# First batch's attention outputs held as fp32 and scaled in the second, and the first loads in another order

## What is computed

```python
# q, k, v: (4, 8, 576, 64)
scores = q @ k.T / 8
mask_local   = (rel >= 0) & (rel < 32)                       # heads 0 to 3
mask_strided = (rel >= 0) & (pos_k % 32 == pos_q % 32)       # heads 4 to 7
attn = softmax(where(mask, scores, -1e9))
x = (attn @ v) as (2304, 512)
h = x @ w_in; g = h * sigmoid(1.702 * h); x = g @ w_out      # 512 -> 2048 -> 512
# then a top-2 mixture of 8 experts (512 -> 1024 -> 512) with noisy gates
```

## Time and profile before

| | us |
|---|---|
| median of 3 runs | 1031.27 |
| lowest, highest | 1027.51, 1045.26 |
| the profiled execution's own time | 1028.2 |
| its span in the trace | 1026.4 |
| TensorE busy | 978.1 (95%) |
| VectorE busy | 594.5 (58%) |
| ScalarE busy | 307.6 (30%) |

### The profile page before, as it was taken

The page is one execution under the profiler, slowest core; times in us unless marked ns, Lnnn a source line. Parts: engine busy times, 40 slices in busy tenths (PEclk is TensorE's granted clock), DMA queues, the critical chain, the costliest instruction groups (busy, mean ns, idle before and its releaser), DMA issues.

```text
span 1026.4 us, 22946 instructions
## 1 busy us (share of the span) xinstructions
PE 978.1 (95%) x9218; PEld 706.8 (69%) x9219; DVE 594.5 (58%) x1033; ACT 307.6 (30%) x427; POOL 219.8 (21%) x274
## 2 busy tenths in 40 slices
PE   7899999999999999999999899989999999999992
PEld 4677777867677576775765767756777767677771
DVE  6588998668777786787887744232232323233231
ACT  2355745523243233332531321111111111111110
POOL 4222323000000000010025124233323333333331
PEclk8699999999999999999999999999999999999997
DMA  9774582097756667567647635848474747475330
GB/s 267 177 187 92 129 196 55 6 393 237 249 204 205 247 214 258 181 205 268 219 149 238 218 78 151 263 114 213 131 210 121 221 120 214 133 209 142 89 82 23
DMA packets 170240, 182.43 MB, mean 178 GB/s; under 512 B 133495, under 2 KB 133495, under 8 KB 167360
## 3 DMA queue, kind: packets, MB, share of 16 engines
q1 hardware_dynamic: 112832, 142.47, 44.6%
q0 software_dynamic: 9600, 27.69, 8.9%
q10 hardware_dynamic: 47744, 11.35, 6.3%
HBM read 116.41 MB, written 53.55 MB: 166 GB/s over the span
## 4 chain that ended last, share of the span: by engine, by line
PE 86%; DVE 4%; DMA 2%; SPq 2%; ACT 2%; issue 1%; POOLq 0%; DVEq 0%; ACTq 0%
PE bank L1760 20%; PE bank L1769 20%; PE bank L1661 18%; PE bank L1586 17%; PE bank L1524 4%; PE bank L1562 3%; PE bank L1494 2%; PE bank L1536 1%; PE bank L1543 1%; PE bank L1513 1%; DMA arena<-out,arena 1%; DMA arena<-in_moe_w 1%; DVE sc L976 1%; SPq L399 1%; ACT arena L725 1%
## 5 line engine op out<-in xcount | busy, mean ns | idle before, releaser
L1586 PE MATMUL bank<-x,w_in_s 128*128 128x256 f16 (+1 forms) x1728 | 194.1, 273 | 2.6 <-DVE x L1021 1.5
L1661 PE MATMUL bank<-w_out_s,arena 128*128 128x512 f16 x864 | 190.2, 379 | 0.0
L1586 PEld LDWEIGHTS bank<-x,w_in_s 128*128 128x128 f16 x1728 | 167.9, 98 | 25.9 <-DVE x L1021 1.8
L1661 PEld LDWEIGHTS bank<-w_out_s,arena 128*128 128x128 f16 x864 | 83.6, 98 | 96.6
L1429 DVE TENSOR_TENSOR arena<-arena 128x512 f32<-128x512 f32 x37 | 25.6, 692 | 161.7 <-ACT arena L899 117.6
L1760 PEld LDWEIGHTS bank<-arena,w_out_s 128*128 128x128 f16 x2016 | 114.5, 98 | 5.9 <-issue 0.8
L1760 PE MATMUL bank<-arena,w_out_s 128*128 128x128 f16 x2016 | 117.0, 219 | 0.6 <-issue 0.6
L1760 PEld LDWEIGHTS bank<-arena,w_in_s 128*128 128x128 f16 x1920 | 109.3, 98 | 5.4 <-issue 0.7
L1760 PE MATMUL bank<-arena,w_in_s 128*128 128x128 f16 x1920 | 111.7, 219 | 0.5 <-issue 0.5
L1769 PE MATMUL bank<-w_out_s,arena 128*128 128x512 f16 x480 | 108.7, 383 | 3.3 <-DVE arena L1424 3.3
L1769 PE MATMUL bank<-w_in_s,arena 128*128 128x512 f16 x480 | 108.6, 383 | 2.3 <-DVE arena L1424 2.3
(11 more groups left out here) (196 smaller groups left out, 992.8 us busy)
## 6 DMA issues: line engine op xcount, KB each, us to landing
arena<-in_moe_w SPq DMA_DIRECT2D x16, 2048.0 KB, 11.5
split_weights<-arena SPq DMA_DIRECT2D x16, 2048.0 KB, 7.4
w_in_s<-split_weights SPq DMA_DIRECT2D x32, 512.0 KB
w_out_s<-split_weights SPq DMA_DIRECT2D x32, 512.0 KB
arena<-in_q SPq DMA_DIRECT2D x32, 144.0 KB, 3.6
arena<-in_k SPq DMA_DIRECT2D x32, 144.0 KB, 3.7
out<-zeros SPq DMA_DIRECT2D x1, 4608.0 KB, 25.1
x_rows<-arena SPq DMA_DIRECT2D x18, 256.0 KB, 3.3
```

What stands on the lines that cost most here:

```text
L1586: last = mm(dst, w_in_s[:, w_part, c, f * P:(f + 1) * P], x1[:, x_part, c, tok], start=(c == 0 and w_part + x_part == 0), stop=(c == DC - ...
L1661: last = mm(ps_x[j], g[par][:, g_part, f, j * P:(j + 1) * P], w_out_s[:, w_part, f], start=(n == 0), stop=(n == 3 * FC - 1))
```

## The change

The outputs of batch 0 are written by `out_hi` as unscaled fp32 into `held_out`, space of `x1` that batches 2 and 3 fill later; DVE has no `out_lo` in stages 0 to 3. In stages 4 to 7 ScalarE and DVE each do one more operation a stage, on 128x576, that scales and splits the held output of the pair with the same hp (`late_hi`, `late_lo`). V's factor is needed in stage 4 instead of stage 0.

Flat V comes in four quarters with a semaphore each: two after the start's first and second transposes, two in SP's iteration 2. `v_max` moves from the start to stages 0, 1 and 2. The V loads of pairs 0 and 1 are started by ScalarE. SP loads q and k of pair i + 2 when pair i's are transposed, and V when pair i - 2's product is done. The maxima of `w_in` are taken in stages 3, 4 and 5 (two in stage 5) instead of 1 to 4, `w_in` is split in stages 7 to 10 instead of 6 to 9, `w_out`'s maxima stay in stages 9 to 12. Between the first transposes and scores stand 14 `busy` products.

```diff
-MAX_IN, SPLIT_IN, MAX_OUT, SPLIT_OUT = 1, 6, 9, 14
+SPLIT_IN, SPLIT_OUT = 7, 14
...
             load_qk(0, 0)
             load_qk(0, 1)
-            sp.dma_start(w_in_s[...], v[0:2] ...).then_inc(S["v_flat_in0"], 16)
-            sp.dma_start(w_out_s[...], v[2:4] ...).then_inc(S["v_flat_in1"], 16)
-            load_v(sp, 0, 0)
-            load_v(sp, 0, 1)
+            sp.wait_ge(S["t_done"], 4)
+            load_qk(0, 2)
+            load_v_flat(0)
+            sp.wait_ge(S["t_done"], 8)
+            load_qk(0, 3)
+            load_v_flat(1)
...
-            for i in range(NPAIR - 2):
-                sp.wait_ge(S["s_done"], i * 2 + 2)
+            for i in range(2, NPAIR - 2):
+                sp.wait_ge(S["t_done"], 8 * i - 2)
                 load_qk((i + 2) // PAIRS, (i + 2) % PAIRS)
+                if i == 2:
+                    for n in (2, 3):
+                        load_v(sp, 0, n)
+                        load_v_flat(n)
+                sp.wait_ge(S["pv_done"], 2 * i - 2)
                 load_v(sp, (i + 2) // PAIRS, (i + 2) % PAIRS)
-                if i < QUARTERS:
+                for n in ([0], [1], [2, 3])[i - 2] if i < 5 else []:
                     c = DC // QUARTERS
-                    wait(sp, S["w_in_in"], 16 * i)
+                    wait(sp, S["w_in_in"], 16 * n)
...
-                n, c = i - SPLIT_IN - 3, FC // QUARTERS
+                n, c = i - SPLIT_IN - 1, FC // QUARTERS
                 if 0 <= n < QUARTERS:
                     sp.wait_ge(S["split_lo"], 2 * n + 2)
                     wait(sp, S["w_out_in"], 16 * n)
...
             def out_hi(b, hp):
                 act.wait_ge(S["pv_done"], i * 2 + 2)
+                if b == 0:
+                    for src, dst in out_views(b, hp, None):
+                        last_op = nc.scalar.activation(dst, src, ACT.Copy)
+                    last_op.then_inc(S["x1_lo"], 1)
+                    return
...
+                if b == 1:
+                    act.wait_ge(S["x1_lo"], 2 + hp)
+                    nc.scalar.activation(x1[:, 0, hp, 0:SEQ], held_out[hp], ACT.Copy, scale=col(S_V)
+                                         ).then_inc(S["late_hi"], 1)
...
             evac_qk(1, 0, 1)
+            load_v(act, 0, 0)
             evac_qk(2, 1, 0)
             evac_qk(3, 1, 1)
             exps(0, 0, 0)
             exps(0, 0, 1)
+            load_v(act, 0, 1)
...
+                if b == 1:
+                    dve.wait_ge(S["late_hi"], hp + 1)
+                    nc.vector.scalar_tensor_tensor(x1[:, 1, hp, 0:SEQ], held_out[hp], col(S_V), x1[:, 0, hp, 0:SEQ],
+                                                   ALU.mult, ALU.subtract).then_inc(S["late_lo"], 1)
...
-            ALL_OF = {0: V_ALL, 1: WG_ALL, MAX_IN + QUARTERS: WI_ALL, MAX_OUT + QUARTERS: WO_ALL}
+            ALL_OF = {PAIRS: V_ALL, SPLIT_IN - 1: WI_ALL, 2 * PAIRS + 2: WG_ALL, SPLIT_OUT - 1: WO_ALL}
...
             transpose_qk(1, 0, 1, 16 * QK_DMAS)
+            busy(2)
             pe.wait_ge(S["consts_pool"], 10)
             scores(0, 0, 0, 2)
+            busy(2)
             scores(0, 0, 1, 2)
+            busy(2)
             transpose_qk(2, 1, 0, 16 * QK_DMAS)
             transpose_qk(3, 1, 1, 16 * QK_DMAS)
+            busy(2)
             scores(0, 1, 0, 4)
+            busy(2)
             scores(0, 1, 1, 4)
+            busy(4)
...
-                        scores(b2, hp2, 0, k[2] + 1,
-                               (V_MAX, 1) if hp == 0 else (B_MAX, b + 2) if hp == 1 else None)
+                        scores(b2, hp2, 0, k[2] + 1, spread)
```

More of the change, by code:

```diff
@@ L312, in program @@
         w_ready = [S["w_even"], S["w_odd"]]
+        v_flat = [t[:].rearrange("p a c f -> p (a c f)").bitcast(F32)[:, 0:HEADS * SEQ] for t in (w_in_s, w_out_s)]
+        held_out = [x1[:, 0, hp, 2 * SEQ:4 * SEQ].bitcast(F32) for hp in range(PAIRS)]
         def is_local(hp):
@@ L337, in out_views @@
         def out_views(b, hp, part):
-            tok = slice(b * SEQ, (b + 1) * SEQ) if isinstance(b, int) else bass.ds(b * SEQ, SEQ)
-            dst = x1[:, part, hp, tok]
+            dst = held_out[hp] if part is None else x1[:, part, hp, b * SEQ:(b + 1) * SEQ]
             if is_local(hp):
@@ L401, in load_qk, with load_v_flat @@
                                      ).then_inc(qk_in[par], 16)
+            def load_v_flat(n):
+                half = HEADS * SEQ // 2
+                at = slice(n % 2 * half, (n % 2 + 1) * half)
+                rows = v[n // 2 * 2:n // 2 * 2 + 2].rearrange("b h (x s) d -> (b h x) (s d)", x=P // (2 * HEADS))
+                sp.dma_start(v_flat[n // 2][:, at], rows[:, at]).then_inc(S[f"v_flat_in{n}"], 16)
             load_qk(0, 0)
             load_qk(0, 1)
[L406 to L411, removed]
-            load_v(sp, 0, 0)
-            load_v(sp, 0, 1)
+            sp.wait_ge(S["t_done"], 4)
[4 more added lines that the diff above has]
+            load_v_flat(1)
             sp.dma_start(wg[:, :, 0:E], w_gate.rearrange("(c p) e -> p c e", p=P)).then_inc(S["small_in"], 16)
@@ L989, in _ @@
             nc.vector.memset(zeros[:], 0.0).then_inc(S["zero_done"], 1)
-            v_flat = [t[:].rearrange("p a c f -> p (a c f)").bitcast(F32)[:, 0:HEADS * SEQ]
-                      for t in (w_in_s, w_out_s)]
+            for c in (V_MAX, B_MAX):
+                nc.vector.memset(col(c), 0.0).then_inc(S["raw_max"], 1)
             def max_and_sub(b, hp, h2, all_of=None):
@@ L1072, in weights @@
             def weights(i):
-                if i == 0:
-                    dve.wait_ge(S["small_in"], 48)
-                    nc.vector.tensor_reduce(col(B_MAX), wg[:], AX.XY, ALU.max, apply_absolute_value=True
-                                            ).then_inc(S["raw_max"], 1)
-                if MAX_IN <= i < MAX_IN + QUARTERS:
-                    weights_max(S["w_in_in"], i - MAX_IN)
+                if i < 3:
+                    v_max(i + 1)
+                if i == 2:
+                    dve.wait_ge(S["step"], steps[0])
+                    absmax(col(V_MAX), col(PART_MAX, 4)).then_inc(S["raw_max"], 1)
+                for n in ([0], [1], [2, 3])[i - 3] if 3 <= i < 6 else []:
+                    weights_max(S["w_in_in"], n)
+                if i == SPLIT_IN:
+                    gate_max()
                 if i == SPLIT_IN - 1:
-                    dve.wait_ge(S["all_max"], 3)
+                    dve.wait_ge(S["all_max"], 2)
                     power_of_two(col(WI_ALL), col(S_WI), col(I_WI), step).then_inc(S["scaled"], 1)
-                if i == 2 * PAIRS:
-                    dve.sem_inc(S["raw_max"], 1)
-                if MAX_OUT <= i < MAX_OUT + QUARTERS:
-                    weights_max(S["w_out_in"], i - MAX_OUT)
+                if SPLIT_IN + 2 <= i < SPLIT_IN + 2 + QUARTERS:
+                    weights_max(S["w_out_in"], i - SPLIT_IN - 2)
                 if i == SPLIT_OUT - 1:
@@ L1107, in stage_a @@
                     if i == 0:
-                        v_max(3)
-                        dve.wait_ge(S["step"], steps[0])
-                        absmax(col(V_MAX), col(PART_MAX, 4)).then_inc(S["raw_max"], 1)
+                        v_max(0)
                     weights_lo(i, 0)
@@ L1610, in stage_a @@
                     b2, hp2 = b + (hp + 2) // PAIRS, (hp + 2) % PAIRS
+                    spread = (V_MAX, b + 2) if hp == 0 and not last else (B_MAX, 2 * b + 2) if hp == 2 else None
+                    if hp == 1 and last:
+                        spread = (B_MAX, 7)
                     loads = (b * 2 + (hp + 2) // 2 + 1) * 16 * QK_DMAS
```

39 lines of the change are left out of this document (21 added, 18 removed).

## The result

| | before | changed |
|---|---|---|
| median us | 1029.39 (1024.59 to 1045.26, 4 runs) | 1072.97 (1069.68 to 1076.59, 4 runs) |
| ratio, 95% interval | | 1.0436 (1.0384 to 1.0487) |
| profiled execution, us | 1028.2 | 1074.63 |
| its span, mean granted clock | 1026.4, 0.976 | 1072.7, 0.934 |

What follows compares the result with a forecast made beforehand. The prediction saw TensorE nearly always busy in stages 1 to 13, so only the half-clock, waiting start could be won: 14.0 - 2.2 - 0.3 - 7.2 = 4.3 us faster, 1028.2 to 1024, range 1016 to 1031.

Steps and rivals of the forecast that it cites:

- rival (b): Clock falls in new gaps, stage 9 likeliest: 5.6 us per fall, one giving 1029.6, two 1035; chance 0.10.
- The price, stage 5: Pair 7's q and k land late behind w_in's quarters on SP's list: stall of 2.2 us taken, 1.2 to 3.5.
- The changed start: Early pair 2 loads and fillers begin stage 0 at 20.5, stage 1 at 30.0 instead of 44.01: 14.0 us gained.
- five stalls: TensorE waits for late q and k: 2.2 us in stage 5; 3.8, 0.6, 1.5 and 1.3 in stages 9 to 12.
- The price, stages 9 to 12: w_out loads wait on later w_in splits, delaying q and k queued behind: 7.2 us, 4.8 to 9.
- DVE's lag: From stage 5 on, DVE assumed one maximum late, 2.3 us, making the w_in splits end later.
- rival (c): Start stays cold: clock still falls at 15.6, stage 1 at 39.8, gain 4.2, total 1031; chance 0.07.
- ScalarE and DVE, 0.3: Stages 4 to 7: added scaling of batch 0's outputs and late copies cost TensorE 0.3 us.
- (a): Loads keep up: no stall in stages 5, 10, 11, smaller in 9 and 12; gain 11 us, 1017; chance 0.23.
- (d): ScalarE held by a 5.91 us V issue at the start, stage 0 3 us later: 1027; chance 0.06.

Runs made afterwards that it cites:

- 12: 9 without the 14 products of the start, one execution: 1012.97 us.
- 16: The kernel of 12 (9 without the 14 products of the start), twelve executions: median 1026.83 us, ratio 0.9913 to the kernel before.
- 7: Kernel before with only the start's part (early pair 2 q and k, ScalarE V loads, 14 products), V's factor still in stage 0: 1031.8 us.
- 2: 1 with w_out's quarters also loaded one SP iteration later: 1043.82 us.
- 10: 9 with pair 5's q and k, and pair 6's, put back behind V of pairs 3 and 4 and w_in's first quarter: 1027.51 us.
- 9: 8 with the spread of w_in's maxima ahead of the second head's scores for hp = 2: median 1017.08 us of 7, ratio 0.9869 to the kernel before.
- 15: 9 with the added products of 3 ahead of each transpose group, four executions: 1016.43 us, ratio 0.988 to the kernel before.
- 5: Changed kernel with SP's loads for pairs 4 to 9 ordered by due time and w_out one iteration later: 1047.44 us.
- 8: 5 with late_hi and late_lo moved into the middle of the next stage, behind the evacuation: 1026.92 us.
- 14: 9 run once more unchanged, for a second profile: 1034.33 us.
- 1: Changed kernel with pair 5's q and k moved ahead of V of pair 3 on SP's list: 1066.8 us.
- 3: 2 with two products of 224 columns ahead of each of a stage's two q and k transpose groups: 1051.68 us.
- 6: 5 with the added products of 3 ahead of each transpose group: 1036.42 us.
- 13: Changed kernel with only the added products of 3 ahead of each transpose group: 1068.28 us.
- 11: 9 with the changed kernel's own SP list whole, w_out included: 1062.57 us.
- 4: Kernel before without the four busy products ahead of each product with V: 1041.25 us.

## Why the prediction was wrong, step by step

**The step that failed is the clock, for which the sum has no term.** It takes every stage at full clock (9.47 and 10.13 us) and leaves a fall to rival (b), at 5.6 us and a chance of 0.10. The changed kernel stood at half clock for 122.6 us of stages 1 to 13, and 49.8 of its 58.8 us there are that. "The price, stage 5" failed beside it: it passed over stage 3, whose stall of 7.67 us was the place of the first fall. The steps in order:

**The changed start: right.** Stage 0 at 20.59 (20.5 forecast), stage 1 at 30.00 (30.0), clock 1.00, ScalarE's issues 0.44 to 0.55 us each. Its reason was only half right: the clock at full speed gives 2 to 3.4 of the 14 us (12, 16), and the step leaned on V's factor having left the path, without which 7 keeps none of them. The prediction worked out from the rule that issuing from a second engine saves little (the Trainium skill, "DMA: Bandwidth & Descriptors", "Issuing engines are not separate DMA queues") that pair 2 would be transposed at 24.4; it was at 21.51. That is not against the rule: SP's list was put in another order too, with pair 2's q and k ahead of V (issued at 7.89 instead of 22.89), and no run here moves the issues to ScalarE alone.

**"The price, stage 5": failed, by what it left out.** It walked down SP's list to pair 7 and asked only there whether the data come in time. Its own numbers had stage 3 on the edge: pair 5's q and k issued from 41.7, behind a quarter of `w_in`, which by its 8.2 us lands them at 49.9, and TensorE wants them at 30.0 + 9.47 + 10.13 + 0.97 = 50.6. A slack of 0.7 us was never written down, though the walk down SP's list rested on six durations taken from elsewhere. Measured, the walk ended at 48.07: pair 4's q and k held SP 6.2 us instead of 2 (one issue pair alone 5.06), pair 4's V 3.8 instead of 2.5, and the quarter's 0.5 was left out. The k landed 10.4 behind the quarter's issue (57.97 - 47.53), not 8.2. So 7.67 us of waiting in stage 3. Stage 5's 2.2 was also too small: with stage 3 mended it is 5.0, and stage 4 has 4.9 beside it (2). What the late pair of stage 3 costs with its fall is 15.6 us (10).

**Rival (b), the clock: right in kind, wrong in price and chance.** It gave a fall 5.6 us, from stage 0 alone, as if the clock came back with the stage. Its rate was right: 5.6 lost in 14.1 us at half is 0.40 for each, against 0.41 and 0.42 measured (0.33 in 10, where some 4 us of the fall lie in the gap). Its length was wrong. The prediction had read the earlier trace rows at 0.50 from 15.6 us and 0.52 up to 44.01, a stretch of over 27 us at half, with TensorE at work for 19.5 of them, and priced only the part from stage 0's q transpose on. In dense work a fall costs 9.0 us when it lasts 27 (10, beside its gap) and 17.2 when it lasts 41 (9 against 15). It was looked for in stage 9 for 3.8 us of gap, and it held "TensorE is dense around each gap" against a fall; in 5, 8, 14 and at the gap of stage 10 a wait of 1.1 to 1.5 us stands right before one. With three falls at 17.2 its sum would have read 1028.2 - 4.3 + 51.6 = 1075.5; the execution took 1074.63. That this comes so near is partly luck: the three lasted 27, 41 and 55 us, and one of them has no gap before it. The chance of 0.10 was too low for a forecast that itself had five stalls.

**"The price, stages 9 to 12": wrong in size.** 3.8, 0.6, 1.5, 1.3 forecast; only stage 10's 1.34 came. The first quarter was issued at 133.96, 3.4 us into stage 8, and the next 2.9 into stage 9, not 6.3: DVE had none of the lag that the step gave it. Stage 8 also lasted 12.5 us instead of 9.47, most of it at half clock, so pair 11's q and k were wanted 3 us later; what these stages would wait at full clock no run shows. That the `w_out` wait with q and k queued behind it is a real price is shown by 1 against 2: 23 us, or 21.4 at stage 14's start, nearly all of it through the falls. (The 4.8 us that the step gives without DVE's lag has terms, 1.9 + 0.3 + 2.1 + 0.5, that don't follow from its bullets; worked through them it is 1.5 + 0.6 + 1.5 + 1.3 = 4.9. In rival (c) 24 + 15.5 is 39.5, not 39.8. Neither moves the forecast.)

**ScalarE and DVE, 0.3: right in the changed kernel** (a wait of 0.51 where 0.25 stands otherwise), and a late copy ahead of the evacuation was named. That DVE's factor of `w_in` comes 1.5 to 2.2 us late once TensorE is at full speed (3, 6, 8, 13) was not: the lag was seen as harmless since "the lag meets the loads first".

**Rivals (a), (c), (d)** fell: the loads didn't keep up, the start wasn't cold, ScalarE wasn't held.

**What stays open.** Why the clock falls in some executions at a strided stage's second transposes with no wait above 0.25 us before it, and not in others of nearly the same kernel, isn't settled: 9's profile has such a fall and 12's, without the 14 products of the start, has none. So the cause of the changed kernel's fall at 97.7, some 17 of its 49.8 us by 0.42 for each microsecond, stays open; that of the other two is shown to be the late loads in so far as 10 brings the first one back and 2 takes the third one away, in one execution each. The kernel before is not free of it either: of its 17 executions beside 16, four took 1050 to 1063 us at a mean clock of 0.926 to 0.955, and none of them has a trace. That the added products keep the clock up is likely (15: four of four executions; 13: the place passed at 1.00), not shown: the executions are few, and five of 9's seven stayed up without them.

## What to carry to other kernels

When an edit pulls the start forward, every later load has less time by the same amount: write down landing and demand for **each** consumer on the issuing engine's list, and treat a slack smaller than the error of the walk as a stall. Where TensorE runs dense small products, price a new gap not by its length but by the clock that it may lose (here 9 to 17 us, behind gaps as small as 1.1 to 1.5, though not behind every one), and mend the list of loads before judging the edit: the same edit took 1062.57 us with one list (11) and 1017.08 with another (9). A gap that is removed uncovers the next one, so look at the whole chain again after each.

## What the runs showed of the hardware

- The clock, once down, stayed at half for 24 to 55 us in most falls, with TensorE busy nearly all the time (39.92 of 40 us, 53.52 of 54), for 10 to 14 us in stage 0 or before it in 7, 12 and 16, and for 3.4 to 7 us in some of 1, 2, 3, 5, 9, 11, 12, 13 and 15. The Trainium skill, page "TensorE: Matmul & The Clock Gate", section "Part 1: The HAM clock gate (the "warmup" mystery)", puts the price of the ramp below 1% of a typical kernel's span. That is said of the warm-up and doesn't cover this kernel, which lost 49.8 of 1072.7 us, 4.6%, because the clock was lost again in mid-kernel.
- It also fell where no wait over 0.25 us stood before it in its stage: in stage 6 in the changed kernel (97.7), 1, 2, 9 and 11, and in stage 10 in 4 and 16, each time as the second q and k transposes of this strided stage began, behind waits of 0.25 and 0.20, and for 37 to 51 us. Three short ones, of 3.4 us, began at the same transposes of a local stage: stage 9 in 5 (waits of 0.25 and 0.20) and stage 13 in 1 and 5 (0.34 and 0.34).
- Two q issues held SP for 5.06 us at 23.28, and in 15 for 4.24 us at the same place and 3.79 at 55.58, where two take 0.86 to 1.38 otherwise. In 7, eight strided V issues at 19.82 took 15.36 us, against 6.4 to 8.5 in the changed kernel. The first loads behind the start's burst are the ones to keep off a critical list.
